# Layer 1's odd chunks squared on ScalarE, and blocks 0 and 1 in different sets of x buffers

## The reference

```
x  = causal mix of 7 tokens, softmaxed weights per head (8 heads of 24 channels)
h  = x @ w1_in                       # 192 -> 2048
g  = h                if h >= 1
     0                if h <= -1
     (h + 1)^2 / 4    between        # layer 1
x  = g @ w1_out                      # 2048 -> 192
h  = x @ w2_in                       # 192 -> 2048
g  = s * relu(h)^2 + b               # layer 2
out = g @ w2_out                     # 2048 -> 192
```

## Time and profile before

| | us |
|---|---|
| median of 3 runs (1148.37 to 1151.63) | 1149.53 |
| the profiled execution, whole | 1150.71 |
| its span, first to last instruction | 1149.0 |
| TensorE busy | 1125.8 (98%) |
| VectorE busy | 947.9 (83%) |
| ScalarE busy | 630.8 (55%) |
| mean granted TensorE clock | 0.993 of full |

### The profile page before, as it was taken

How to read it: one execution, slowest core, us unless ns; L and a number is a source line. 1 busy time by engine, 2 the same in 40 slices (tenths; PEclk the granted TensorE clock), 3 DMA queues, 4 the chain that set the end, 5 groups by cost and what they waited for, 6 DMA issues and landing times.

```text
span 1149.0 us, 23218 instructions
## 1 busy us (share of the span) xinstructions
PE 1125.8 (98%) x9746; PEld 951.0 (83%) x9746; DVE 947.9 (83%) x858; ACT 630.8 (55%) x627; POOL 3.4 (0%) x16
## 2 busy tenths in 40 slices
PE   5999999999999999999999999999999999999998
PEld 3777878888888888888888888888888888888886
DVE  7998998978888798888888798887888878866665
ACT  4545655555565655555555555555555555565544
POOL 1000000000000000000000000000000000000000
PEclk8998999999999999999999999999999999999999
DMA  6002300100001000000000000000000000000000
GB/s 183 1 1 65 93 1 1 29 29 1 1 1 29 28 1 1 1 29 28 1 2 1 29 29 1 1 1 29 29 1 2 1 29 1 1 1 1 29 1 28
DMA packets 12423, 21.33 MB, mean 19 GB/s; under 512 B 1073, under 2 KB 5169, under 8 KB 12337
## 3 DMA queue, kind: packets, MB, share of 16 engines
q1 hardware_dynamic: 12256, 19.99, 6.1%
q0 software_dynamic: 64, 0.00, 0.0%
q10 hardware_dynamic: 16, 0.00, 0.0%
HBM read 13.70 MB, written 6.29 MB: 17 GB/s over the span
## 4 chain that ended last, share of the span: by engine, by line
PE 88%; DVE 8%; issue 3%; ACT 1%; DMA 0%; SPq 0%; DVEq 0%; ACTq 0%
PE acc L717 28%; PE h L670 23%; PE h L683 18%; PE acc_rem L732 18%; DVE g L445 3%; DVE g L453 1%; DVE mixed L502 1%; DMA xraw_rem<-in_x 0%; ACT g_hi L303 0%; DVE mixed_rem L516 0%; DVE mixed L516 0%; DVE up_lo L551 0%; DVE up_rem_lo L551 0%; DVE g_lo L463 0%; DVE dn_lo L551 0%
## 5 line engine op out<-in xcount | busy, mean ns | idle before, releaser
L303 ACT ACTIVATE g_hi<-g 128x1024 fp32r<-128x1024 f32 x128 | 135.8, 1061 | 218.8 <-DVE g L453 218.7
L447 DVE SCALAR_TENSOR_TENSOR g<-r,scale,h 128x1024 f32<-128x1024 f32 x128 | 161.9, 1278 | 69.5 <-ACT r L291 69.5
L305 ACT ACTIVATE g_hi<-g,shift 128x1024 fp32r<-128x1024 f32 x128 | 147.6, 1153 | 116.5 <-PE acc_rem L732 101.4
L717 PE MATMUL acc<-g_hi,dn_hi 64*128 64x512 f32 x1024 | 204.7, 389 | 0.4 <-issue 0.4
L732 PE MATMUL acc_rem<-g_lo,dn_rem 64*128 64x512 f32 x1024 | 204.6, 388 | 0.0
L732 PE MATMUL acc_rem<-g_hi,dn_rem 64*128 64x512 f32 x1024 | 204.6, 387 | 0.0
L717 PE MATMUL acc<-g_lo,dn_hi 64*128 64x512 f32 x1024 | 204.3, 388 | 0.0
L717 PE MATMUL acc<-g_hi,dn_lo 64*128 64x512 f32 x1024 | 204.0, 387 | 0.0
L466 DVE SCALAR_TENSOR_TENSOR g_lo<-g,shift,g_hi 128x1024 fp32r<-128x1024 f32 x128 | 164.1, 1282 | 43.6 <-ACT g_hi L305 43.4
L463 DVE TENSOR_TENSOR g_lo<-g,g_hi 128x1024 fp32r<-128x1024 f32 x128 | 156.8, 1225 | 42.9 <-ACT g_hi L303 42.7
L291 ACT ACTIVATE r<-h 128x1024 f32<-128x1024 f32 x128 | 128.1, 1026 | 109.6 <-PE h L683 97.5
(11 more groups left out here) (96 smaller groups left out, 1356.4 us busy)
## 6 DMA issues: line engine op xcount, KB each, us to landing
xraw<-in_x SPq DMA_DIRECT2D x7, 518.0 KB, 4.3
out<-res SPq DMA_DIRECT2D x7, 512.0 KB, 3.3
stage<-in_moe_w_out SPq DMA_DIRECT2D x6, 384.0 KB, 3.4
xraw_rem<-in_x SPq DMA_DIRECT2D x14, 129.5 KB, 4.0
out<-res_rem SPq DMA_DIRECT2D x7, 256.0 KB, 3.6
stage<-in_moe_w_in SPq DMA_DIRECT2D x2, 512.0 KB, 5.4
stage<-in_moe_w_in SPq DMA_DIRECT2D x4, 256.0 KB, 5.1
xraw<-in_x SPq DMA_DIRECT2D x1, 512.0 KB, 4.2
```

The source lines that it names most:

```text
L303: nc.scalar.activation(g_hi[k][:], g[k][:], ACT.Copy).then_inc(hi_ready, 1)
L305: nc.scalar.activation(g_hi[k][:], g[k][:], ACT.Identity, bias=shift[:, 0:1]).then_inc(hi_ready, 1)
L447: nc.vector.scalar_tensor_tensor(g[k][:], r[k][:], scale[:, 0:1], h[k][:], ALU.mult, ALU.mult).then_inc(h_used, 1)
L717: last = nc.tensor.matmul(acc[:, t, :], w[rows], v[rows, t, :], start=(j == 0 and side == 0 and n == 0), stop=(j == CH - 1 and side == 1 a ...
```

## The change

1. For odd chunks of layer 1, in every phase of layer 1, `second` goes. ScalarE squares r in place (`square_odd`, behind a wait for its own relu), and VectorE's `first` becomes g = min(max(h, 1), r^2) in one instruction. `round_g` of an odd chunk waits for `h_used` in place of `g_ready`. Even chunks stay.
2. Block 0 uses X2 in place of X1, so X1 is free all through phase 0.
3. Block 1 is mixed in chunks 1 to 12 (before: 1 to 14) and split into X1 in chunks 8, 9, 13 and 14 (before: behind first(15)).

```
 def relu(layer, S, k):
...
     if layer == 0:
-        nc.scalar.activation(r[k][:], h[k][:], ACT.Relu, scale=0.5, bias=half[:, 0:1]).then_inc(r_ready, 1)
+        nc.scalar.activation(r[k][:], h[k][:], ACT.Relu, scale=0.5,
+                             bias=half[:, 0:1]).then_inc((r_ready, odd_relu_done)[k], 1)
...
+def square_odd(count):
+    act.wait_ge(odd_relu_done, count)
+    nc.scalar.activation(r[1][:], r[1][:], ACT.Square).then_inc(r_ready, 1)
...
 def round_g(layer, S, k, g_count):
-    if layer == 0:
+    if layer == 0 and k == 0:
         act.wait_ge(g_ready, g_count)
     else:
         act.wait_ge(h_used, S + 1)
...
     # ScalarE's phase
     relu(layer, S0 + j, j % 2)
+    if layer == 0 and j % 2:
+        square_odd(G0 + j // 2 + 1)
...
-phase(0, None, 0, 0, 0, extras={n - 4: [lambda n=n: weights_hi(0, n)] for n in range(5, 8)},
-      last=[lambda: round_mixed(1, X1, CH - 1), lambda: round_mixed_rem(1, X1, CH - 1)])
+e = {n - 4: [lambda n=n: weights_hi(0, n)] for n in range(5, 8)}
+e[8] = [lambda: round_mixed_rem(1, X1, None)]
+e[13] = [lambda: round_mixed(1, X1, None)]
+phase(0, None, 0, 0, 0, extras=e)
...
 # VectorE's first
-if layer == 0:
+if layer == 0 and k == 0:
     nc.vector.tensor_tensor(g[k][:], h[k][:], r[k][:], ALU.max).then_inc(h_used, 1)
+elif layer == 0:
+    nc.vector.scalar_tensor_tensor(g[k][:], h[k][:], 1.0, r[k][:],
+                                   ALU.max, ALU.min).then_inc(h_used, 1)
...
-    if layer == 0:
-        second(S0 + j, j % 2)
+    if layer == 0 and j % 2 == 0:
+        second_even(S0 + j)
...
-e = mixing(1, lambda part, k: TAPS * part + k + 1)
+e = mixing(1, lambda part, k: 6 * part + max(1, k))
 for n in (5, 6, 7):
     e[n - 4].append(lambda n=n: weights_lo(0, n))
-phase(0, None, 0, 0, extras=e, last=[lambda: low_mixed(1, X1), lambda: low_mixed_rem(1, X1)])
+e[9].append(lambda: low_mixed_rem(1, X1))
+e[14] = [lambda: low_mixed(1, X1)]
+phase(0, None, 0, 0, extras=e)
...
 # TensorE
-phase(0, None, 0, 0, X1, first_split, weights)
+phase(0, None, 0, 0, X2, first_split, weights)
```

More of the change, by code:

```diff
@@ L135, in build @@
         r_ready = sem("r_ready")
+        odd_relu_done = sem("odd_relu_done")
         h_used = sem("h_used")
@@ L358, in weights_hi, with phase @@
                     nc.scalar.activation(hi, cols, ACT.Copy).then_inc(w_hi_done, 1)
-            def phase(layer, before, S0, P0, G0, blk_before=None, extras=None, last=None):
+            def phase(layer, before, S0, P0, G0=None, blk_before=None, extras=None, last=None):
                 for j in range(CH):
@@ L366, in phase @@
                         if before is not None:
-                            round_g(before, S0 - 1, 1, G0)
+                            round_g(before, S0 - 1, 1, None)
                     elif j % 2 == 0:
-                        round_g(layer, S0 + j - 1, (j - 1) % 2, G0 + j)
+                        round_g(layer, S0 + j - 1, 1, None)
                     relu(layer, S0 + j, j % 2)
+                    if layer == 0 and j % 2:
+                        square_odd(G0 + j // 2 + 1)
                     if j == CH - 1:
@@ L374, in phase @@
                     if j % 2:
-                        round_g(layer, S0 + j - 1, (j - 1) % 2, G0 + j)
+                        round_g(layer, S0 + j - 1, 0, G0 + j // 2 + 1 if layer == 0 else None)
                     if j == 1 and before is not None:
@@ L393, in _ @@
             act.wait_ge(mixed_pe_done, 1)
-            nc.scalar.activation(X1[0][:, 1, :], mixed_pe, ACT.Copy).then_inc(mixed_pe_hi, 1)
+            nc.scalar.activation(X2[0][:, 1, :], mixed_pe, ACT.Copy).then_inc(mixed_pe_hi, 1)
             act.wait_ge(mix_step, 2 * TAPS)
-            nc.scalar.activation(X1[0][:, 0, :], mixed[:, 0, :], ACT.Copy).then_inc(x_hi_done[0], 1)
-            round_mixed_rem(0, X1, None, interleaved=True)
+            nc.scalar.activation(X2[0][:, 0, :], mixed[:, 0, :], ACT.Copy).then_inc(x_hi_done[0], 1)
+            round_mixed_rem(0, X2, None, interleaved=True)
             for n in range(2, 5):
@@ L406, in _ @@
             e[13] = [lambda: round_y_rem(0, X2, None)]
-            phase(0, 0, CH, 1, CH, blk_before=0, extras=e)
+            phase(0, 0, CH, 1, CH // 2, blk_before=0, extras=e)
             act.wait_ge(scalars_loaded, 32)
@@ L412, in _ @@
                 S1, P1 = S0 + CH, P0 + 1
-                phase(1, 0, S0, P0, (c + 2) * CH, blk_before=c + 1, extras={
+                phase(1, 0, S0, P0, blk_before=c + 1, extras={
                     6: [lambda: round_mixed_rem(c + 2, X1, S0 - 1)],
                     12: [lambda: round_mixed(c + 2, X1, S0 - 1)]})
-                phase(0, 1, S1, P1, (c + 2) * CH, blk_before=c, extras={
+                phase(0, 1, S1, P1, (c + 2) * (CH // 2), blk_before=c, extras={
                     4: [lambda: round_y(P0 - 1, X2, S1 - 1)],
@@ L420, in _ @@
             S0, P0 = (LOOPS + 1) * 2 * CH, (LOOPS + 1) * 2
-            phase(1, 0, S0, P0, NB * CH, blk_before=NB - 1, extras={
+            phase(1, 0, S0, P0, blk_before=NB - 1, extras={
                 4: [lambda: round_y(P0 - 1, X1, S0 - 1)],
                 8: [lambda: round_y_rem(NB - 1, X1, S0 - 1)]})
-            phase(1, 1, S0 + CH, P0 + 1, NB * CH, blk_before=NB - 2)
+            phase(1, 1, S0 + CH, P0 + 1, blk_before=NB - 2)
             round_g(1, S0 + 2 * CH - 1, 1, None)
@@ L448, in first, with second_even @@
                                                    ALU.mult, ALU.mult).then_inc(h_used, 1)
-            def second(S, k):
+            def second_even(S):
                 dve.wait_ge(h_used, S + 1)
-                nc.vector.scalar_tensor_tensor(g[k][:], r[k][:], 1.0, g[k][:],
+                nc.vector.scalar_tensor_tensor(g[0][:], r[0][:], 1.0, g[0][:],
                                                ALU.min, ALU.mult).then_inc(g_ready, 1)
@@ L608, in _ @@
             dve.wait_ge(mixed_pe_hi, 1)
-            nc.vector.tensor_tensor(X1[1][:, 1, :], mixed_pe, X1[0][:, 1, :].bitcast(F32),
+            nc.vector.tensor_tensor(X2[1][:, 1, :], mixed_pe, X2[0][:, 1, :].bitcast(F32),
                                     ALU.subtract).then_inc(mixed_pe_lo, 1)
             dve.wait_ge(x_hi_done[0], 1)
-            nc.vector.tensor_tensor(X1[1][:, 0, :], mixed[:, 0, :], X1[0][:, 0, :].bitcast(F32),
+            nc.vector.tensor_tensor(X2[1][:, 0, :], mixed[:, 0, :], X2[0][:, 0, :].bitcast(F32),
                                     ALU.subtract).then_inc(x_lo_done[0], 1)
             weights_lo(0, 1)
-            low_mixed_rem(0, X1)
+            low_mixed_rem(0, X2)
             for n in range(2, 5):
```

## The result

The changed kernel takes 1140.43 us (median of 4 runs, 1139.75 to 1140.6) against 1149.76 (4 runs, 1148.37 to 1151.63). The ratio is 0.9917, 95% interval 0.9900 to 0.9934: 9.3 us faster. Two more sets of runs on other chips gave 0.9910 (0.9897 to 0.9924) and 0.9919 (0.9905 to 0.9932). The forecast was 1139.1. The profiled executions are 1150.71 and 1139.75, their spans 1149.0 and 1138.0; the 11.0 us between them are what the traces explain.

A forecast was written before the change was run, and what follows sets the result against it. TensorE, 98% busy, was taken as the bound, with 12.5 us lost before the loop. Gains of 3.9 (phase 0), 4.4 (seam) and 2.1 (phase 1) sum to 10.4 us; off the 1149.53 median, 1139.1 us, range 1137.0 to 1141.5.

The forecast's parts named there:

- A: Stage from up_own(3)'s first step to phase 1's first step: 261 steps, 5.5 us lost by TensorE.
- B: Stage of phase 1's first 15 steps: 4.4 us lost, mostly slow clock behind a wait.
- C: Stage from phase 1's 16th step to the third phase's 11th: 299 steps, 2.6 us lost.
- The square: ScalarE's added pass in odd layer 1 chunks: 1.05 to 1.15 us each, hidden, worth 0 in the loop.
- the walk: Chunk-by-chunk timing of phases 0 and 1 and the seam from instruction spacings, giving gains of 3.9, 4.4 and 2.1 us.
- Phase 0: Walk of stage A: two gaps stay, 0.75 + 0.1 and 0.65 + 0.1 us; gain 3.9 us.
- The seam: Start of phase 1, stage B: block 1's x ready in time, no wait or slow clock; gain 4.4 us.
- Phase 1: Stage C: odd-chunk gaps go, 0.5 us of loss stays; gain 2.1 us.
- Rival 1: Phase 0: VectorE still sets the pace; gain only 7.5 us, 1142 us; chance 0.11.
- Rival 2: Seam or chunks 8 to 11: a wait of 1 us or more brings the low clock; gain 6.4, 1143; chance 0.06.
- Rival 3: Seam: new order of chunks 8 to 14 comes too late, x_lo waits; gain 5.5 us, 1144; chance 0.03.
- Rival 4: ScalarE: each square switches the table and back, delaying first(odd); slower, 1170 or 1260 us; chance 0.04.

The follow-up runs named there:

- The square alone: Only odd-chunk squaring on ScalarE added to the kernel before; block 0 stays in X1, mixing in chunks 1 to 14, splits behind first(15): 1146.36 us, ratio 0.9929.
- the x sets alone: Kernel before with block 0 in X2 and block 1 mixed and split inside phase 0; odd chunks keep `second` on VectorE: 1153.94 us, ratio 0.9994.
- the fills: Changed kernel with VectorE's two splits back behind first(15) and one or two idle VectorE passes ahead of them: 0.9934 and 0.9959 of the kernel before.
- one pass more: Changed kernel with one extra ScalarE copy of r in place between square and first(odd): 1154.03 us, 0.9990 of the kernel before.
- Two passes more: Changed kernel with two extra ScalarE copies of r in place between square and first(odd): 1202.17 us, 1.0420 of the kernel before.

## Why the prediction was right

Point by point, by its own steps.

- **The bound.** Right: all of the gain lies ahead of the third phase, and the loop is as full as before. Of the 12.5 us that TensorE lost in A, B and C, 2.05 are left.
- **The square.** Costed at 1.05 to 1.15 against 1.062 measured, the new `first` at 1.22 against 1.219. Its value of 0 in the loop is shown by the same step lengths and no idle time. But the walk looked at a plain pair only. In two of eight pairs first(odd) does wait for the square, 0.56 and 0.92 us, and only the slack behind it keeps TensorE from noticing. In the pair about 260 us the square runs to 262.29 and first(odd) starts at 262.62, behind second(even), as the walk had it:

```profile
261.23 1.06 ACT L298 ACTIVATE r<-r 128x1024 f32<-128x1024 f32 x1
261.48 1.23 DVE L467 SCALAR_TENSOR_TENSOR g<-r,g 128x1024 f32<-128x1024 f32 x1
262.62 1.22 DVE L458 SCALAR_TENSOR_TENSOR g<-h,r 128x1024 f32<-128x1024 f32 x1
```

- **VectorE's relief** was put at 78 us; it is 71.8. The sum took durations (1.22), where back-to-back instructions start 1.13 apart: 64 x 1.13 = 72.3. The walk itself used 1.13 and is not touched.
- **Phase 0.** Both gaps came where the walk put them: 0.83 + 0.11 lost near 39.8 (forecast 0.75 + 0.1) and 0.74 + 0.11 near 75.3 (0.65 + 0.1). A won 3.6 of 3.9 forecast; the 0.3 are these and steps that run some hundredths over 0.2273 all through the stage.
- **The seam.** 4.4 forecast, 4.4 measured. But the reason was given too simply. I credited the 4.4 to x being ready early. The square alone already brings B from 4.4 lost to 2.0: its seam's first wait is shorter (0.79 lost in place of 1.76) and in its trace the clock holds. The early splits are worth the other 2.0 in B and the 0.79 ahead of it, which stands in A. The crowding of chunks 1 to 3, 8 and 9 takes some 0.8 of that back (0.76 of it near 76 us in the trace on that chip), and 0.7 more went to the low clock behind 30 us, which I put down to chance. With the square in place the x sets bring 1.4 us by the medians (1146.36 to 1144.94, ranges that just overlap), not 4.4.
- **Phase 1.** 2.5 against 2.1. The 0.5 that I kept for low_y_rem ahead of first(15) is 0.1: the slack of 0.16 held. This is all the square's: the x sets alone lose 3.2 there.
- **Rival 1** (VectorE sets the pace) is true of the x sets alone, at 97% busy. With the change VectorE is busy 94.5% of stage A (57.04 of 60.36; the prediction had 92) and still makes the two gaps, but A keeps 1.95, not 3.5. **Rival 2** did not come; the fills show that its mechanism exists. **Rival 3** did not come: x_lo's pass runs at 91.98 without a wait. **Rival 4**: one table load, no switch. Its threshold of 1.8 us of delay was too high: one pass more, some 0.8 us of delay in a plain pair and 1.1 in the pairs with extras on ScalarE, already costs 6 us in the loop and nearly the whole gain. Its sum has a slip as well: 2.3 us later against 1.6 of slack leaves 0.7 a plain pair, not 0.3, so by its own terms it should have been some 16 us above 1170. Two passes more show the step itself: plain pairs there lose 0.4 each, with first(odd) held up by 1.85 us. And the chances given for slower and same (0.05 each) do not add up from the cases: 0.04 and half of 0.06 make 0.07 and 0.03.

The median came 1.3 us over the forecast: the 11.0 us of the two profiled executions are 9.3 in the medians, since the profiled one of before lay 1.0 above its median and the changed one's 0.7 below.

## What to carry to other kernels

Where the bottleneck engine is full in the loop, look at the ends: count its steps per stage, price each stage against the loop's step, and the loss has an address before anything is changed. Move work off the engine that paces the short stages to one that has room, and check that the moved pass is hidden behind what the old engine does meanwhile, in the pair with the most extras and not in the plain one. When two edits serve one seam, run each alone: here one of them did most of both.

## What the runs showed of the hardware

- In one trace each, TensorE's granted clock went to its lower level (0.43 us a step in place of 0.227) behind waits that lost 1.38 and 1.21 us close together, and stayed at the upper one through 0.79, 0.63 and 1.21 in 3.6 us, and through 0.21 and 1.21. A fall at the seam cost 1.7 to 2.5 us on top of the waits. The same wait in the same kernel (1.77 us, at 28 to 31 us) was followed by the lower level in two traces and not in a third, so one trace does not tell what a wait costs.
- The steady step of the changed kernel was 0.2273 us on two chips and 0.2286 on a third, the same through 13 phases (69.07 and 69.43 us each). On a fourth, layer 2 phases took 69.07 us in one kernel's trace and 69.43 in another's, and that first kernel ran once at 1149.60, the run of the trace, and nine times at 1153.80 to 1155.57. The two step lengths are 5 us apart over the run, half of what the change brings: kernels are to be compared with several runs each on one chip.
- A ScalarE pass over 128x1024 float32 in place took 1.062 us for Square as for Copy, a VectorE pass with max and min between PSUM and SBUF 1.219, no more than a plain one.
